# A fused mixing and two-layer kernel: one load of mixing weights goes ahead of the second layer's weight loads, and the preparation of those weights moves to later chunks

## The reference

```python
w = softmax(weight_gen, axis=-1)                 # (2, 4096, 8 heads, 7 taps), sum + 1e-9
x1[b, s, h*24 + g] = sum_k w[b, s, h, k] * x_pad[b, s + k, h*24 + g]     # d_model = 192
h  = x1 @ moe_w_in                                # 192 -> 2048
P  = a0 + a1*h + a2*h^2 + a3*h^3
Q  = 1 + |b0|*|h| + |b1|*h^2
x2 = (P / (Q + 1e-6)) @ moe_w_out                 # 2048 -> 192
h  = x2 @ moe2_w_in                               # 192 -> 2048
y  = (h * clip(h + 3, 0, 6) / 6) @ moe2_w_out     # 2048 -> 192
```

## Time and profile before

| | us |
|---|---|
| median of 3 runs | 1242.54 (1242.28 to 1243.18) |
| the profiled execution's own time | 1243.18 |
| its span | 1241.4 |
| TensorE busy | 1197.4 (96%) |
| VectorE busy | 1170.6 (94%) |
| ScalarE busy | 1169.6 (94%) |
| GpSimd busy | 1133.7 (91%) |

### The profile page before, as it was taken

How to read it: one execution, slowest core, us unless ns; L and a number is a source line. 1 busy time by engine, 2 the same in 40 slices (tenths; PEclk the granted TensorE clock), 3 DMA queues, 4 the chain that set the end, 5 groups by cost and what they waited for, 6 DMA issues and landing times.

```text
span 1241.4 us, 19302 instructions
## 1 busy us (share of the span) xinstructions
PE 1197.4 (96%) x5211; PEld 975.5 (79%) x5211; DVE 1170.6 (94%) x1884; ACT 1169.6 (94%) x2197; POOL 1133.7 (91%) x892
## 2 busy tenths in 40 slices
PE   6676999999999999999999999999999999999998
PEld 5444788888888888888888888888888888888876
DVE  8899999999999999999999999999999999999933
ACT  6888999999999999999999999999999999999954
POOL 7999899999999999999999999999999999966664
PEclk9989999999999999999999999999999999999999
DMA  8863132233313233321322333122333212010000
GB/s 202 170 148 64 42 77 52 60 73 81 68 42 75 55 75 73 73 60 40 89 58 60 73 79 68 39 70 64 68 73 73 60 48 47 14 22 22 5 22 18
DMA packets 64774, 80.79 MB, mean 65 GB/s; under 512 B 15832, under 2 KB 42200, under 8 KB 64408
## 3 DMA queue, kind: packets, MB, share of 16 engines
q1 hardware_dynamic: 63464, 77.59, 27.1%
q0 software_dynamic: 1200, 1.97, 1.4%
HBM read 57.49 MB, written 9.98 MB: 54 GB/s over the span
## 4 chain that ended last, share of the span: by engine, by line
PE 90%; DVE 4%; ACT 2%; issue 2%; DMA 1%; POOL 1%; DVEq 0%; SPq 0%; ACTq 0%
PE h L750 9%; PE acc L757 9%; PE acc L767 9%; PE acc L764 9%; PE acc L761 9%; PE acc L758 9%; PE h L751 9%; PE h L752 9%; PE h L753 9%; PE h L754 9%; DMA late<-in_moe_w_in 1%; DVE early L1261 1%; DVE early L1255 1%; PE h L774 1%; DVE q_recip L1269 1%
## 5 line engine op out<-in xcount | busy, mean ns | idle before, releaser
L683 POOL TENSOR_TENSOR g_lo<-late,g_hi 128x512 fp32r<-128x512 f32 x255 | 344.2, 1350 | 60.8 <-ACT g_hi L1034 40.6
L673 POOL TENSOR_TENSOR g_lo<-early,g_hi 128x512 fp32r<-128x512 f32 x256 | 345.5, 1350 | 1.7 <-ACT g_hi L1011 1.6
L750 PE MATMUL h<-x_hi,w_in_hi 128*128 128x512 f32 x511 | 202.7, 397 | 21.6 <-DVE early L1285 20.7
L1293 DVE SCALAR_TENSOR_TENSOR late<-late,h 128x512 f32<-128x512 f32 x256 | 174.3, 681 | 42.1 <-ACT late L1022 40.6
L764 PE MATMUL acc<-g_lo,w_out 128*128 128x512 f32 x512 | 200.4, 391 | 1.7 <-POOL g_lo L673 1.7
L757 PE MATMUL acc<-g_hi,w_out 128*128 128x512 f32 x512 | 199.7, 390 | 0.8 <-DVE x_lo L1299 0.7
L767 PE MATMUL acc<-g_lo,w_out 128*128 128x512 f32 x512 | 200.0, 391 | 0.0
L761 PE MATMUL acc<-g_hi,w_out 128*128 128x512 f32 x512 | 199.9, 390 | 0.0
L758 PE MATMUL acc<-g_hi,w_out 128*128 128x512 f32 x512 | 199.8, 390 | 0.0
L751 PE MATMUL h<-x_lo,w_in_hi 128*128 128x512 f32 x511 | 199.5, 390 | 0.0
L752 PE MATMUL h<-x_hi,w_in_lo 128*128 128x512 f32 x511 | 199.3, 390 | 0.0
(11 more groups left out here) (115 smaller groups left out, 2414.0 us busy)
## 6 DMA issues: line engine op xcount, KB each, us to landing
mix_w<-mix_weights SPq DMA_DIRECT2D x75, 192.0 KB
mix_w<-mix_weights SPq DMA_DIRECT2D x75, 144.0 KB
x_win<-in_x SPq DMA_DIRECT2D x15, 393.0 KB, 3.2
mix_w<-mix_weights SPq DMA_DIRECT2D x60, 96.0 KB
mix_w<-mix_weights SPq DMA_DIRECT2D x60, 72.0 KB
late<-late SPq DMA_DIRECT2D x32, 128.0 KB, 2.3
out_y<-late SPq DMA_DIRECT2D x16, 256.0 KB, 2.0
x_tail_hi<-tail_hi SPq DMA_DIRECT2D x60, 64.0 KB, 2.0
```

What stands on the lines that cost most here:

```text
L673: nc.gpsimd.tensor_tensor(g1_lo[p][:, :], neg_g[p], g1_hi[p][:, :].bitcast(F32), ALU.subtract).then_inc(g1_lo_ready, 1)
L683: nc.gpsimd.tensor_tensor(g2_lo[p][:, :], gate[p], g2_hi[p][:, :].bitcast(F32), ALU.subtract).then_inc(g2_lo_ready, 1)
L750: pe.matmul(out[:, :], w_hi[:, cols], hi[:, :], start=True, stop=False)
```

## The change

The SP list of segment -1 stores mixing part 1 and loads the second half of block 1's mixing weights before it loads w_in2 (tail and main). Casts and splits of w_in2, and those of w_out2, go to other chunks. The reciprocals of part 1 move from n = 2 to 3, its scaling from 5 to 4. Of the four maxima of part 2, which lay in c = 3, 4, 5, 6 of segment 0, one is now in c = 3, two are in 5 and one is in 7.

```diff
@@ -328,11 +328,11 @@
 
 
 
-        IN_HI = {6: ((1, 0),), 7: ((1, 1),), 8: ((1, 2), (1, 3),)}
-        TAIL_HI = {7: ((1, 0),), 8: ((1, 1),), 9: ((1, 2),), 10: ((1, 3),)}
-        OUT_HI = {1: ((0, 0),), 3: ((0, 1),), 5: ((0, 2),), 7: ((0, 3),), 9: ((1, 0),), 10: ((1, 1),), 11: ((1, 2),), 16: ((1, 3),)}
-        OUT_LO = {2: ((0, 0),), 6: ((0, 1),), 7: ((0, 2),), 10: ((0, 3),), 13: ((1, 0), (1, 1),), 16: ((1, 2),), 19: ((1, 3),)}
-        EXP_1, SUM_1, RECIP_1, SCALE_1 = 1, 1, 2, 5
+        IN_HI = {11: ((1, 0),), 15: ((1, 1),), 16: ((1, 2),), 17: ((1, 3),)}
+        TAIL_HI = {10: ((1, 0),), 11: ((1, 1),), 13: ((1, 2),), 14: ((1, 3),)}
+        OUT_HI = {1: ((0, 0),), 3: ((0, 1),), 5: ((0, 2),), 7: ((0, 3),), 13: ((1, 0),), 14: ((1, 1),), 18: ((1, 2), (1, 3),)}
+        OUT_LO = {2: ((0, 0),), 6: ((0, 1),), 7: ((0, 2),), 10: ((0, 3),), 15: ((1, 0),), 17: ((1, 1),), 20: ((1, 2),), 21: ((1, 3),)}
+        EXP_1, SUM_1, RECIP_1, SCALE_1 = 1, 1, 3, 4
 
         IN1_HI = {2: (2,), 3: (3,)}
         IN1_LO = {4: (2, 3,)}
@@ -360,7 +360,7 @@
 
         EARLY_STEPS = {"max": {4: (0,), 5: (1, 2,), 12: (3,)}, "sub": {13: (0,)}}
         LATE_STEPS = {"exp": {1: (0,)}, "sum": {2: (1,), 7: (2, 3, 4, 5,), 9: (6, 7,)}, "recip": {12: (0, 1,)}, "scale": {13: (0,)}}
-        THIRD_EARLY = {"max": {3: (0,), 4: (1,), 5: (2,), 6: (3,)}, "sub": {8: (0,)}, "exp": {9: (0,)}, "sum": {10: (1,), 11: (2,), 12: (3, 4, 5,), 13: (6, 7,)}, "recip": {14: (0, 1,)}}
+        THIRD_EARLY = {"max": {3: (0,), 5: (1, 2,), 7: (3,)}, "sub": {8: (0,)}, "exp": {9: (0,)}, "sum": {10: (1,), 11: (2,), 12: (3, 4, 5,), 13: (6, 7,)}, "recip": {14: (0, 1,)}}
         THIRD_LATE = {"scale": {1: (0,)}}
 
         def part_steps(s, step, c):
@@ -469,13 +469,13 @@
             sp.wait_ge(gen_stored[0], 16)
             load_mix_w(1, slice(0, A_TAPS), mix_w_a)
             sp.dma_start(w_slot(out_slot[1]), w_half(w_out1, 1)).then_inc(out1_staged[1], 16)
-            load_tail(1, w_in2, slice(0, F), in2_tail_staged)
-            sp.wait_ge(in1_lo, 4)
-            sp.dma_start(in_slot, w_in2[0:P, :]).then_inc(in2_staged, 16)
             sp.wait_ge(gen_scaled, 2)
             store_gen(1)
             sp.wait_ge(gen_stored[1], 16)
             load_mix_w(1, slice(A_TAPS, K), mix_w_b)
+            load_tail(1, w_in2, slice(0, F), in2_tail_staged)
+            sp.wait_ge(in1_lo, 4)
+            sp.dma_start(in_slot, w_in2[0:P, :]).then_inc(in2_staged, 16)
 
             def mix_done(blk, taps):
```

## The result

The kernel after took 1245.09 us in the median of 19 runs (1244.57 to 1246.27), the kernel before 1243.26 us in 19 runs beside them (1242.28 to 1245.92). The ratio is 1.0013 with a 95% interval of 1.0007 to 1.0019: the change costs 1.6 us (0.9 to 2.4). That is more than chance, but under the 0.2% that the forecast took as the bound for a difference. The forecast was 1243.9 us, +1.4 on the median shown then. The profiled execution of after took 1244.64 us with a span of 1242.8, and 1244.6 was worked out for it.

What follows compares the result with a forecast made beforehand. Before TensorE's endless run at 127.36 us, GpSimd, ScalarE and VectorE share the bound; the rest is fixed. Terms -2.2, +3.7 and -0.1 give +1.4 us on the 1242.54 median: 1243.9 us, range 1241.0 to 1246.4.

Steps and rivals of the forecast that it cites:

- Up to n = 8, nothing.: First layer-1 chunks: removing ScalarE's 3.6 us stall is worth almost zero, since quotients still wait for g_lo from GpSimd.
- n = 8 to 13: Layer-1 chunks: 3.9 us lead at n = 12, cut to 2.2 by ScalarE's wait for GpSimd's last mixing addition.
- n = 13 to 19: Layer-1 chunks: five uncovered VectorE splits (3.0) and ScalarE's casts (+1.2), less 0.5 of small waits, give +3.7 us.
- n = 19 to the mark: From chunk 19 to TensorE's back-to-back matmuls (the mark): -0.1 us; part 2's load and GpSimd's moved work stay hidden.
- the 1 us in hand: Between n = 19 and the mark: about 1 us of slack before the quotient that needs the later g_lo(18).
- The sum.: -2.2 up to n = 13, +3.7 to n = 19, -0.1 up to the mark: +1.4 us in all.
- Gain: ScalarE's wait at n = 12 and casts at 13, 14 cost less: at most 2.5 us won, middle -1.7; chance 0.24.
- GpSimd at n = 20 to 22: Two w_out2 pairs delay g_lo(18) if n = 16 starts on GpSimd after 86.5: +2.7 us; chance 0.12.
- Late w_in2: w_in2 lands after 70 us and ScalarE stalls at n = 11; landing at 76 adds 2 us; chance 0.02.
- Clock: One more fall of TensorE's clock behind n = 14 costs 1.2 us, +2.6 in all; chance 0.09.

Runs made afterwards that it cites:

- experiment 6: Kernel after with ScalarE's first two casts of w_out2 moved from n = 13 and 14 to n = 9 and 10: 1245.05 us, 1.0014.
- experiment 4: Kernel after with part of one mixing tap left out, about 3 us off GpSimd's list, output incomplete: 1242.82 us, 0.9993.
- the hybrids: Two kernels with w_in2's tail loaded and cast early, its main rows behind the mixing weights; second loads w_out2's second half later: 1243.50 and 1242.46 us.
- the version that won: Second of the hybrids, w_out2's second-half casts moved to n = 15 and 17, its first split to n = 16: 1241.68 us, 0.9988 to before.
- experiments 2: Kernel before with only casts, splits and maxima in their new chunks; load order, reciprocals and scaling as before: 1246.16 us, 1.0021.
- 5: Kernel after with filler matmuls added on TensorE, 10 at n = 7 and 8 at n = 8: 1245.19 us, 1.0018.
- 7: Kernel after with three unused 128x512 operations on VectorE at n = 7: 1245.23 us, 1.0013.
- 10: Second of the hybrids: the first with w_out2's second half loaded behind block 1's tail copies, its casts and splits later: 1242.46 us, 0.9998.
- 11: The version that won, also the last one built: 1241.68 us, 0.9988.
- experiment 9: Kernel after with one unused 128x512 subtraction on VectorE beside each main split at n = 16, 17 and 18: 1247.06 us, 1.0030.
- the first hybrid: Kernel with w_in2's tail loaded early, main rows behind the mixing weights, tail and main casts back at n = 6 to 11: 1243.50 us, 1.0006.

## Why the prediction was right

*Up to n = 8, nothing.* Right. D(8) = 56.44 (forecast 56.5); the quotients wait 2.05 and 2.79 us for g_lo, and the unused operations at n = 7 were free. The removed stall was worth 0.4 us at n = 8, and it takes both reliefs, of ScalarE and of GpSimd, to get more: with GpSimd alone relieved D(7) stayed at 51.38. The store was issued at 36.54 as worked out (36.6), but landed in 2.4 us, not in the 7.9 taken as the bound, so w_in2's main rows landed at 57.7, ahead of my 60 to 66. Nobody needed them then.

*n = 8 to 13.* Right at its end, with an error in between that was taken up, which is luck. D(9) to D(12) came 0.4 to 0.6 us later than forecast: quotient(7) waited for g_lo until 60.75, not 60.5, and I had overlooked that TensorE at half clock (49 to 61 us) makes ScalarE wait, 1.46 us until 59.17. But ScalarE had to stand for the tail cast anyway (2.04 us at 76.29; forecast 76.2), which took it up: D(13) = 79.57 for 79.5. The run with the unused operations at n = 7 shows the same from the other side: D(9) = 61.25 and D(12) = 73.83 were 0.4 and 0.3 us earlier than in after, D(13) = 79.48 only 0.1.

The wait is not the only thing that takes the lead there. I had priced chunk 12 by ScalarE alone, but it carries two splits, and VectorE without a wait takes 5.21 us for it (74.65 to 79.86 in experiment 6, 71.74 to 76.95 in experiment 4) where before took 4.06. From 74.15 that gives 79.36, so of the 1.4 us of lead lost between n = 12 and 13 the splits alone would have cost 1.15 and the wait adds 0.2. The prediction says that all moved splits lie where nothing else is late; that holds for five of the eight, and its sum rightly charges five. Three lie at n = 11 and 12, ahead of this wait.

*n = 13 to 19.* D(14) 84.62, D(15) 89.24, D(17) 98.22, D(19) 107.15 against 84.6, 89.2, 98.3, 107.2. The price of a moved split behind the shadow was confirmed by doubling three of them (+1.55 us at n = 19, 0.52 each, where I had 0.55). What I had not seen is that n = 14 has a second chain as long as ScalarE's.

*n = 19 to the mark.* The load of part 2 was issued at 106.47 (forecast 106.7) and landed in 2.6 us; its maximum stood at 110.92 with no wait. The prediction worked out 2.5 us for it from the Trainium skill (DMA: Bandwidth & Descriptors, Anatomy of one DMA); the 2.6 measured agrees, though that section is about DMAs that GpSimd issues and this one is SP's. g_lo(18) ended at 118.60, just past the 117.4 to 118.4 given, and the 1 us in hand was not there: TensorE waited 0.86 us for it. The lag at n = 22 and 23 was 1.53 and 1.26 us all the same, about that of n = 19 (1.45). Mark 128.89 for 128.8.

*The sum.* Its three terms were -2.2, +3.7 and -0.1; measured at D(13), from there to D(19), and from there to the mark, they are -2.1, +3.5 and +0.1. In all +1.4 forecast; +1.53 at the mark, +1.46 between the two profiled executions, +1.83 between the medians and 1.6 by the ratio. The rest of the 1.2 us by which the median (1245.09) lies above the 1243.9 is the base: the kernel before has 1243.26 in 19 runs, not 1242.54.

*The rivals.* Gain: GpSimd's idle time did not fall but rose by 1.8 us. GpSimd at n = 20 to 22: the g_lo that stood at 86.96 started at 85.62, on the early side of the 86.5 at which that rival decided; the hybrids, which reach n = 19 earlier, do run into it. Late w_in2: no wait. Clock: neither profiled execution of after has a fall at a costly place; whether some of its other runs have one, and whether that makes the 0.2 to 0.4 us between profile and medians, stays open.

## What to carry to other kernels

A stall that ends first in a shadow (here ScalarE's 3.6 us behind GpSimd's g_lo) is worth next to nothing when removed, but the shadow itself is worth something: work placed in it is free, and a change that frees the engine earlier by moving that work behind the shadow pays for all of it. Before moving work, write down for each chunk who ends last and who is second; the second is what a relief of the first uncovers, as at n = 12 and 14 and in the hybrid. When several engines take turns, look at where the one with the longest list (GpSimd) idles up to the mark, and what could fill that: the version that won was the one that idled least, though over all versions the idle time did not order the times.

## What the hardware showed that I had not expected

TensorE's granted clock falls at differing places from one profiled execution to the next between 87 and 127 us, in kernels with nearly the same list: none in before or in the first profile of after, one at 108.17 to 111.02 in the second profile of after, two with the filler matmuls (107.1 to 110.6 and 121.11 to 124.10), one at 118.41 to 121.40 in the last version. Its price depends on the place. The step D(23) - D(22) is 4.37 us in after, without a fall there. In seven executions a fall lies inside that chunk or begins just ahead of it: in six of them (experiments 2, 4, 5, 7, 10 and 11; the last two with other tables) the step is 4.97 to 5.32 us, 0.6 to 0.95 more, and in the seventh (experiment 9) 4.62, 0.25 more. The second profile of after had its fall in n = 19 and lost nothing:

```profile
125.24 0.74 DVE L1249 SCALAR_TENSOR_TENSOR early<-early,coef,h 128x512 f32<-128x512 f32 x1
```

That is D(23) where the first profile had 125.31. I had written that any fall between 107 and 125 us would cost 1.1 us; that was wrong.

The landing time of a DMA was a matter of what stood ahead of it more than of its size: the store of 224 KB took 7.8 us in before, behind the w_in2 loads, and 2.4 in after, ahead of them; a 64 KB copy took 7.0 us in the first hybrid and 2.0 in the second, where the 768 KB load stood behind it.
